# First batch of an FFT and two MLPs in one kernel: the rows of B that token tile 0 needs get a store and loads of their own

## Reference

```python
X = np.fft.rfft(x, axis=1)
y = np.fft.irfft(X * (filt_r + 1j * filt_i), n=3008, axis=1)      # 4 x 3008 x 256
h = y.reshape(12032, 256) @ moe_w_in
z = np.maximum(h, 0) ** 2 @ moe_w_out
g = z @ moe2_w_gate
out = (g / (1 + np.exp(-g)) * (z @ moe2_w_val)) @ moe2_w_out
```

## Time and profile before

| | us |
|---|---|
| median of 3 runs | 2359.86 (2359.42 to 2360.5) |
| the profiled execution, its own time | 2358.64 |
| its span in the profile | 2356.8 |

### The profile page before, as it was taken

The page is one execution under the profiler, slowest core; times in us unless marked ns, Lnnn a source line. Parts: engine busy times, 40 slices in busy tenths (PEclk is TensorE's granted clock), DMA queues, the critical chain, the costliest instruction groups (busy, mean ns, idle before and its releaser), DMA issues.

```text
span 2356.8 us, 31292 instructions
## 1 busy us (share of the span) xinstructions
PE 2329.5 (99%) x10581; PEld 1903.6 (81%) x10581; DVE 1601.1 (68%) x2707; ACT 1272.7 (54%) x2468; POOL 61.2 (3%) x124
## 2 busy tenths in 40 slices
PE   8899999999999999999999999999999999999999
PEld 4688888888888888888888878888888888888887
DVE  3567766677666776566555777777777777777776
ACT  4566656566655665555544445555555555555554
POOL 0100000000000000000000000000000000000000
PEclk9899999999999999999999999999999999999999
DMA  9643433333333333101002101001011011010000
GB/s 270 207 132 96 129 96 107 91 107 112 101 98 99 99 106 122 29 27 42 27 19 72 50 1 36 23 14 36 1 36 36 1 36 36 1 36 28 10 19 18
DMA packets 95423, 153.74 MB, mean 65 GB/s; under 512 B 10080, under 2 KB 48416, under 8 KB 94976
## 3 DMA queue, kind: packets, MB, share of 16 engines
q1 hardware_dynamic: 82112, 132.96, 17.9%
q0 software_dynamic: 13152, 18.78, 3.3%
HBM read 101.89 MB, written 49.81 MB: 64 GB/s over the span
## 4 chain that ended last, share of the span: by engine, by line
PE 96%; DMA 2%; SPq 1%; ACT 1%; issue 1%; DVE 1%; POOL 0%; ACTq 0%; DVEq 0%
PE psum L1450 31%; PE psum L1452 31%; PE psum L1451 31%; PE psum L1552 1%; DMA filt0b<-filt 1%; PE psum L1554 1%; PE psum L1461 1%; DMA B_scratch<-b_out 0%; SPq L562 0%; SPq L557 0%; PE psum L1504 0%; DMA w<-w_full 0%; ACT turned L820 0%; DMA A_scratch<-a_out 0%; ACT z_raw L820 0%
## 5 line engine op out<-in xcount | busy, mean ns | idle before, releaser
L1217 DVE SCALAR_TENSOR_TENSOR prod<-psum,act_out 128x512 f32<-128x512 f32 (+1 forms) x384 | 260.9, 679 | 398.4 <-ACT act_out L917 397.9
L917 ACT ACTIVATE act_out<-psum 128x512 f32<-128x512 f32 (+1 forms) x384 | 226.1, 589 | 461.5 <-PE psum L1452 461.2
L1450 PE MATMUL psum<-g_hi,m_hi 128*128 128x512 f32 (+1 forms) x768 | 305.7, 398 | 2.0 <-ACT z_raw L820 1.8
L1450 PE MATMUL psum<-v_hi,m_hi 128*128 128x512 f32 (+1 forms) x768 | 297.7, 388 | 1.5 <-DVE v_lo L1115 1.5
L1452 PE MATMUL psum<-v_hi,m_lo 128*128 128x512 f32 (+1 forms) x768 | 296.7, 386 | 0.0
L1451 PE MATMUL psum<-v_lo,m_hi 128*128 128x512 f32 (+1 forms) x768 | 296.7, 386 | 0.0
L1452 PE MATMUL psum<-g_hi,m_lo 128*128 128x512 f32 (+1 forms) x768 | 296.5, 386 | 0.0
L1451 PE MATMUL psum<-g_lo,m_hi 128*128 128x512 f32 (+1 forms) x768 | 296.4, 386 | 0.0
L1115 DVE TENSOR_TENSOR g_lo<-prod,g_hi 128x512 fp32r<-128x512 f32 (+1 forms) x408 | 270.6, 663 | 1.1 <-ACT g_hi L820 1.0
L820 ACT ACTIVATE g_hi<-prod 128x512 fp32r<-128x512 f32 (+1 forms) x408 | 248.5, 609 | 0.9 <-DVE prod L1251 0.9
L1450 PE MATMUL psum<-g_hi,m_out 128*128 128x512 f32 (+1 forms) x576 | 226.0, 392 | 0.3 <-DVE g_lo L1115 0.3
(11 more groups left out here) (125 smaller groups left out, 4246.9 us busy)
## 6 DMA issues: line engine op xcount, KB each, us to landing
filt_in<-filt SPq DMA_DIRECT2D x36, 512.0 KB, 3.9
z_scratch<-z_raw SPq DMA_DIRECT2D x23, 512.0 KB, 2.9
b_in<-B_scratch SPq DMA_DIRECT2D x122, 96.0 KB, 2.8
zq_raw<-z_scratch SPq DMA_DIRECT2D x44, 256.0 KB, 3.5
B_scratch<-b_out SPq DMA_DIRECT2D x38, 256.0 KB, 2.1
A_scratch<-a_out SPq DMA_DIRECT2D x50, 192.0 KB, 2.1
x_in<-x SPq DMA_DIRECT2D x48, 192.0 KB, 2.8
a_in<-A_scratch SPq DMA_DIRECT2D x36, 256.0 KB, 3.3
```

What stands on the lines that cost most here:

```text
L917: nc.scalar.activation(act_out[n % 2][:, 0:w], psum[:, n % 3, 0:w], ACT.Relu).then_inc(relu_done, 1)
L1217: nc.vector.scalar_tensor_tensor(out=prod[n % 2][:, 0:w], in0=psum[:, n % 3, 0:w], scalar=0.0, in1=act_out[n % 2][:, 0:w], op0=ALU.max, op ...
L1450: nc.tensor.matmul(dst, wh, vh, start=start, stop=False, skip_group_check=True)
```

## The change

Each pair of B of batch 0 is divided. The columns of the matrix `inv` of the table `w23_full` are put in another order, so that the 24 rows that tile 0 needs (4 groups x 6 rows) come out on the partitions 0 to 23, and the other 104 rows behind them. The two parts go to two tensors of their own in HBM, `B0_here_d` (stored by SP) and `B0_rest_d` (stored by POOL, now for all 12 pairs). SP's loop over the pairs is: store the 24 rows of pair u, then load those of pair u - 1 with two DMAs of 24 KB. `copy_b0` waits for both stores of its buffer. The 7 matmuls of `keep_busy` ahead of `s4_0` become 13. In `up1(0)` the wait for `v_lo` is divided by half c.

```diff
@@ -94,7 +94,9 @@
     turn = np.concatenate([-sign, sign])[:, None]
-    w23_full = np.concatenate([fwd, swapped, inv, turn], 1)
+    rows = np.arange(P).reshape(P // NP, NP)
+    first = np.concatenate([rows[:, 0:PAIR * G0].reshape(-1), rows[:, PAIR * G0:].reshape(-1)])
+    w23_full = np.concatenate([fwd, swapped, inv[:, first], turn], 1)
     return [np.ascontiguousarray(v, dtype=np.float32) for v in (w1, w4, w23, w1_full, w4_full, w23_full)]
@@ -132,7 +134,11 @@
     A_d = nc.dram_tensor("A_scratch", [B, K2, P, D], F32, kind="Internal").ap()
-    B_d = nc.dram_tensor("B_scratch", [B, UPS, P, PAIR, D], F32, kind="Internal").ap()
+    R = P // NP
+    HERE, REST = PAIR * G0, NP - PAIR * G0
+    B0_here_d = nc.dram_tensor("B0_here_scratch", [UPS, R * HERE, PAIR, D], F32, kind="Internal").ap()
+    B0_rest_d = nc.dram_tensor("B0_rest_scratch", [UPS, R * REST, PAIR, D], F32, kind="Internal").ap()
+    B_d = nc.dram_tensor("B_scratch", [B - 1, UPS, P, PAIR, D], F32, kind="Internal").ap()
     z_d = nc.dram_tensor("z_scratch", [TILES, P, CH, T], F32, kind="Internal").ap()
@@ -306,9 +312,8 @@
         b0_stored = [sem(f"b0_stored{k}") for k in range(4)]
+        b0_here_stored = [sem(f"b0_here_stored{k}") for k in range(4)]
         b0_loaded = sem("b0_loaded")
-        b0_last_stored = [sem(f"b0_last_stored{k}") for k in range(2)]
-        b0_last_loaded = sem("b0_last_loaded")
         s4_0_done = sem("s4_0_done")
@@ -485,9 +490,11 @@
-        def b_rows(b, k):
-
-            return B_d[b, :, :, k, :].rearrange("u (r p) d -> (u r) p d", p=NP)
+        def b_rows(b, k, lo, hi):
+
+            if b == 0:
+                return B0_rest_d[:, :, k, :].rearrange("u (r p) d -> (u r) p d", p=REST)[:, lo - HERE:hi - HERE, :]
+            return B_d[b - 1, :, :, k, :].rearrange("u (r p) d -> (u r) p d", p=NP)[:, lo:hi, :]
@@ -561,23 +568,16 @@
-            def store_last_b0(u):
+            def store_b0_here(u):
                 sp.wait_ge(b0_copied, u + 1)
-                sp.dma_start(B_d[0, u], b0_out[u % 4][:, :, :]).then_inc(b0_last_stored[u % 2], 16)
-
-            def load_b0(n):
-                for u in (2 * n, 2 * n + 1):
-                    sp.wait_ge(b0_stored[u % 4], 16 * (u // 4 + 1))
+                sp.dma_start(B0_here_d[u], b0_out[u % 4][0:R * HERE, :, :]).then_inc(b0_here_stored[u % 4], 16)
+
+            def load_b0(u):
+                sp.wait_ge(b0_here_stored[u % 4], 16 * (u // 4 + 1))
                 for k in range(PAIR):
-                    sp.dma_start(b0_in[16 * n + k:16 * (n + 1):PAIR, :, :],
-                                 b_rows(0, k)[8 * n:8 * (n + 1), 0:PAIR * G0, :]).then_inc(b0_loaded, 16)
-
-            def load_last_b0():
-                for h in range(2):
-                    sp.wait_ge(b0_last_stored[h], 16)
-                for k in range(PAIR):
-                    sp.dma_start(b0_in[ROWS - 16 + k:ROWS:PAIR, :, :],
-                                 b_rows(0, k)[ROWS // 2 - 8:, 0:PAIR * G0, :]).then_inc(b0_last_loaded, 16)
+                    rows = slice(PAIR * R * u + k, PAIR * R * (u + 1), PAIR)
+                    sp.dma_start(b0_in[rows, :, :], B0_here_d[u, :, k, :].rearrange("(r p) d -> r p d", p=HERE))\
+                      .then_inc(b0_loaded, 16)
@@ -613,7 +613,7 @@
                 sp.wait_ge(b_copied, u + 1)
-                sp.dma_start(B_d[b + 1, k], b_out[u % 2][:, :, :])\
+                sp.dma_start(B_d[b, k], b_out[u % 2][:, :, :])\
                   .then_inc(b_stored[u % 2], 16)
@@ -621,15 +621,13 @@
                     for h in range(4):
-                        sp.wait_ge(b0_stored[h], 16 * -(-(UPS - 2 - h) // 4))
-                    for h in range(2):
-                        sp.wait_ge(b0_last_stored[h], 16)
+                        sp.wait_ge(b0_stored[h], 16 * UPS // 4)
                 elif i == 0:
                 for k in range(PAIR):
-                    sp.dma_start(b_in[g % 2][k:ROWS:PAIR, :, :], b_rows(b, k)[:, PAIR * i:PAIR * (i + 1), :])\
+                    sp.dma_start(b_in[g % 2][k:ROWS:PAIR, :, :], b_rows(b, k, PAIR * i, PAIR * (i + 1)))\
                       .then_inc(b_loaded[g % 2], 16)
@@ -724,13 +722,12 @@
             load_w_out(0)
-            for n in range(UPS // 2 - 2):
-                load_b0(n)
-            store_last_b0(UPS - 2)
-            load_b0(UPS // 2 - 2)
-            store_last_b0(UPS - 1)
-            load_last_b0()
-            sp.wait_ge(b0_last_loaded, 16 * PAIR)
+            for u in range(UPS):
+                store_b0_here(u)
+                if u:
+                    load_b0(u - 1)
+            load_b0(UPS - 1)
+            sp.wait_ge(b0_loaded, 16 * PAIR * UPS)
             for k in range(1, 4):
@@ -786,7 +783,7 @@
                 pool.wait_ge(b0_copied, u + 1)
-                pool.dma_start(B_d[0, u], b0_out[u % 4][:, :, :]).then_inc(b0_stored[u % 4], 16)
+                pool.dma_start(B0_rest_d[u], b0_out[u % 4][R * HERE:, :, :]).then_inc(b0_stored[u % 4], 16)
@@ -802,7 +799,7 @@
-            for u in range(UPS - 2):
+            for u in range(UPS):
                 store_b0(u)
@@ -835,6 +832,7 @@
                     act.wait_ge(b0_stored[u % 4], 16 * (u // 4))
+                    act.wait_ge(b0_here_stored[u % 4], 16 * (u // 4))
                 copy(flat(b0_out[u % 4][:, :, :]), psum[:, 3 * (u % 2) + 2, :]).then_inc(b0_copied, 1)
@@ -1496,8 +1494,7 @@
                     pe.wait_ge(b0_copied, UPS)
-                    pe.wait_ge(b0_loaded, 16 * (UPS - 2))
-                    pe.wait_ge(b0_last_loaded, 16 * PAIR)
+                    pe.wait_ge(b0_loaded, 16 * PAIR * UPS)
                 for n in range(PAIR * G0):
@@ -1571,12 +1568,14 @@
                 w, col = WIDTH[t], T * t % RING
-                if f == 0:
+                if f == 0 and t:
                     pe.wait_ge(v_lo_done, v_count[t])
                 for c in range(CH):
+                    if n == 0:
+                        pe.wait_ge(v_lo_done, c + 1)
                     last = product(psum[:, n % 3, 0:w], (w_in1(m1_hi, c, f), w_in1(m1_lo, c, f)),
@@ -1701,7 +1700,7 @@
             s3_0(UPS - 1)
-            keep_busy(7)
+            keep_busy(13)
             for c in range(CH):
```

## The result

The changed kernel takes 2373.02 us (median of 5 runs, 2371.75 to 2379.89), the kernel before beside it 2359.42: ratio 1.0067, 95% interval 1.0051 to 1.0084. By the medians it is slower by 13.6 us (the ratio is taken over all runs, of which two of the changed kernel took 2377 and 2380 us, and says 16); the forecast was 2367, 7 us slower, with a range of 2360 to 2375. The sign and the stall behind the small stores came as forecast; the forecast size was half of what came, and the clock behaved otherwise than forecast. The profiled execution has a span of 2371.2 us, 14.4 more than before.

What follows compares the result with a forecast made beforehand. It took the last rows of B reaching s4_0, then b_in's landing before TensorE's x_lo, as the limits; 2358.64 + 7.8 - 0.7 = 2365.7, or 2367 on the median's footing, range 2360 to 2375 us.

Steps and rivals of the forecast that it cites:

- the queue: SP's first small store, issued at 50.5, stands behind SP's earlier transfers and lands at 61.0; TensorE stalls 7.5 us.
- SP's loop: Store and two loads per pair, 1.91 us by issue; store 11 at 79.6, later than its copy at 76.0.
- TensorE's rest: Rival 1: with loads issued in 0.44 us, TensorE's remaining work sets the end, s4_0 at 81.4, 2363.2 us; chance 0.15.
- S: Start of s4_0, the matmul behind the last rows of B: 77.45 before, forecast 85.2, so +7.8 us.
- Rival 3: Small stores land in 2.4 us from the start, the edit works as it reads: 2358.8 or 2353.7 us; chance 0.12.
- Rival 2: No queue behind the weights: first small store lands at 57.4, s4_0 at 86.1, time 2368 us; chance 0.08.
- Rival 5: Fillers don't hold the clock because s4_0 comes over 5 us behind them: 0.7 us dearer; no separate chance given.
- the bound of T with nothing freed: T: first small store's landing, when pair 4's copy can run; forecast 61.0, bound 64.3 if no POOL traffic is freed.
- POOL's tables: Table loads come behind the last copy, at about 77, landed by 82, needed 14 us after S: put at nothing.
- The last landing: Store 11 issued 79.6, landed 82.0, last load behind it; collision with tables would add one landing, 2 to 3 us.
- The cover behind S: Up to b_in's landing 12.7 us after S, 5.5 us of faster work stay hidden; only -0.7 us reaches the end.
- the clock stays at 2.4 GHz: Thirteen fillers, 75.3 to 84.0, end 1.2 us before S and hold the clock; s4_0 takes 2.7 instead of 5.4 us.

Runs made afterwards that it cites:

- weights_mid: The changed kernel, but SP issues the first two weight pieces (1 MB) in its loop behind the loads of pair 3: 2376.22 us, ratio 1.0069 to before.
- pool_both: The changed kernel, but POOL issues both stores of each pair and SP only loads: 2362.22 us, ratio 1.0009 to before.
- act_store: The changed kernel, but ScalarE issues the 24-row store right behind its copy and SP only loads: 2362.53 us, ratio 1.0014 to before.
- tables_late: The changed kernel, but POOL issues its tables (1 MB) only when the last rows of B are in: 2375.78 us, ratio 1.0065 to before.
- before_x_b: The kernel before, but SP issues the first two x_in and first b_in ahead of the 3 MB of weights: 2359.15 us, ratio 1.0001.
- fill7: The changed kernel with 7 fillers in keep_busy instead of 13: 2372.69 us, ratio 1.0048 to before.

## Why the prediction was right and wrong

Right: the queue. The first small store waited for what SP had issued before it, `weights_mid`, `pool_both` and `act_store` show it, and TensorE stood from 55.5 to 61.9 (forecast 54.1 to 61.6), with the clock falling in it. That the first landing came at 61.1, where 61.0 was forecast, is in part luck. The sum was 64.0 less 3.0 for stores of POOL that go missing. In the execution, SP issued its last weight piece at 45.84, 1.3 us earlier than before; the piece needed 15.9 us and not 16.9; and the small store landed 0.7 us ahead of it:

```profile
m_raw<-m_weights SPq DMA_DIRECT2D x1, 512.0 KB, 15.9
```

So at most 1.0 of the 3.0 us can be put down to the missing stores. SP's loop, not TensorE's rest, set S: the copy of pair 11 ran at 75.50 (forecast 75.4), the last store was issued 6.4 us behind it. Rival 3, the edit working as it reads, has its condition, landings under 3 us at 50 us, in no kernel here in SP's queue. Rival 2 is refuted by the landing at 61.1 (it had 57.4) and by the three kernels named. Rival 5 came true: S came 5.95 us behind the fillers and they didn't hold the clock, which the rival had priced at 0.7 us. Two figures of the working are off without moving the forecast: the bound of T with nothing freed is 64.0, not 64.3, and 61.6 + 11.7 + 2.3 is 75.6, not 75.3.

Wrong in size, by four terms of the sum; the step that failed most is POOL's tables, put at nothing. Against 7.1 the spans differ by 14.4:

- *SP's loop.* The pitch was taken as 1.91 us, bound by issue, with landings of 2.4. It was (81.89 - 62.56)/9 = 2.15: +2.1 us. Of these 1.6 go with the tables (1.97 us in `tables_late`); the last two turns of the change, beside the tables, took 2.55 and 2.64 us. The rest, 0.5 us, is landings not short enough in every turn (3.26 us in one on the chain) or issue; the two were not separated.
- *The last landing.* I wrote that the tables would be behind the last copy and named "one landing" as the price of a collision, and left it out of the sum at nothing. The last copy is not the last store: SP was 6 us behind, the tables (issued from 76.94) met its last stores, and S came 7.0 us after store 11 and not 5.6: +1.4 us. In `tables_late` it was 5.3. So the tables, at nothing in the sum, cost 3.3 us of the 3.7 by which S was missed; 0.2 us more came from T and the issue of store 2.
- *The cover behind S.* Forecast -0.7, measured +0.9. The fillers ended 5.95 us before S and not 1.2, and the clock fell 2.5 us after their end, where the earlier trace rows showed 5.0 for the gap of before; I took that one gap for a constant. So "the clock stays at 2.4 GHz" failed, and `s4_0` took 5.40 us, not 2.7. And the last part of b_in landed 1.5 us later behind S: it was issued at the same distance (4.2 us) but needed 9.4 us from its issue, with the instruction fetch among the transfers. +1.6 us.
- *The clock behind the gap.* After 4.2 us of standing the clock was at half for another 3.4 us, a loss of 1.7 us, which no term had. The kernel before stood for 1.9 us there and kept 2.4 GHz. That the longer gap is the cause is not shown: `before_x_b` lost the same behind 1.80 us.

Together 2.1 + 1.4 + 0.2 + 1.6 + 1.7 = 7.0, and 7.1 + 7.0 = 14.1 of the 14.4. The claim that the 5.5 us of clock and split wait can't reach the end held in `act_store`, whose `s1` came 1.3 us earlier; but its reason was half right. b_in's landing is the limit as soon as S or the clock improves; in the kernel before, the order on ScalarE and VectorE was as late as b_in, which its chain and `before_x_b` show.

What stays open: why the clock fell 2.5 us after the last work in one gap and 5.0 in another, and why it is at half behind some gaps of 1.8 us and not behind others. And the fetch: that it moves and that b_in moves with it is shown, but that the fetch by itself makes the late part, and what it is worth at the end, was not tried apart from the fillers.

## What to carry to other kernels

A transfer's place in its issuer's queue is part of its price: before a small store gets a wait that others stand behind, look at what the same engine has issued in the last 15 us, and give the store to a queue that is empty. Where a term is set to nothing because something else is later, work out by how much, with the change's own delays in it. And a faster stretch pays only up to the next landing: here the kernel was faster (0.9982) only with both limits gone.

## What the runs showed of the hardware

One engine's DMA queue holds a small transfer back while another engine's doesn't: a 48 KB store issued by SP at 48 to 53 us landed after 11.5 to 13.7 us, at most 0.7 us before or 0.2 us behind the last of SP's earlier transfers, and POOL's twelve, issued from 42.5 to 68.5 us, landed after 2.8 to 7.7 us. A 1 MB load of tables by POOL, in flight beside SP's last small stores, made their landings 4.99 us for 2.50. Instructions are fetched by the same DMA engines, and six fillers more ahead of a burst were enough to move a 16 KB fetch into it. TensorE's granted clock was at 0.50 for some 3.4 us behind a gap of 1.80 us in `before_x_b`, and stayed at 1.00 behind 2.91 us in `fill7`. An issue of the same small store took 0.46 us on SP, 0.52 on POOL and 0.30 on ScalarE.
